# Masked attention of a three-stage kernel: q and k split and hashed in pairs of heads, the exponential before the casts, and VectorE taking the next row extreme before the remainders

## The reference

```
mask = q_bucket[..., :, None] == k_bucket[..., None, :]
scores = where(mask, q @ k.T / sqrt(64), -1e9)
attn = exp(scores - rowmax); attn /= sum(attn) + 1e-9
x = attn @ v                                   # (1536, 512) over both batches
P = sinkhorn(x @ w_gate)                       # 8 experts, soft
x = sum_e P[:, e] * (relu(x @ w1[e]) @ w2[e])  # every token, every expert
out[n] = gate[n] * (relu(x[n] @ v1[e(n)]) @ v2[e(n)])   # one expert for each token
```

## Time and profile before

| | us |
|---|---|
| median of 3 runs (lowest, highest) | 1681.65 (1680.28, 1683.01) |
| the profiled execution | 1685.06 |
| span of its core | 1683.4 |

### The profile page before, as it was taken

How to read it: one execution, slowest core, us unless ns; L and a number is a source line. 1 busy time by engine, 2 the same in 40 slices (tenths; PEclk the granted TensorE clock), 3 DMA queues, 4 the chain that set the end, 5 groups by cost and what they waited for, 6 DMA issues and landing times.

```text
span 1683.4 us, 21614 instructions
## 1 busy us (share of the span) xinstructions
PE 1592.0 (95%) x7588; PEld 1311.0 (78%) x7589; DVE 666.2 (40%) x1227; ACT 505.3 (30%) x943; POOL 305.0 (18%) x380
## 2 busy tenths in 40 slices
PE   7999998899999999999999999999999991789997
PEld 6888887688888888888888888888888871667775
DVE  7999998442211211211311311221122144554223
ACT  5887877311111110111111111111112133553123
POOL 3333342400020120030030030030030004422102
PEclk9999999999999999999999999999999995899999
DMA  4343343200110110110110020020020015653310
GB/s 137 92 122 91 107 122 124 101 1 1 50 51 0 51 50 0 50 50 0 50 50 0 12 88 0 0 100 0 0 87 14 1 51 178 228 204 130 116 40 22
DMA packets 49381, 108.07 MB, mean 64 GB/s; under 512 B 7350, under 2 KB 13494, under 8 KB 49344
## 3 DMA queue, kind: packets, MB, share of 16 engines
q1 hardware_dynamic: 44208, 96.30, 17.2%
q0 software_dynamic: 2400, 6.31, 1.0%
q10 hardware_dynamic: 2736, 4.98, 1.0%
HBM read 81.58 MB, written 13.40 MB: 56 GB/s over the span
## 4 chain that ended last, share of the span: by engine, by line
PE 80%; DVE 7%; issue 5%; ACT 3%; DMA 3%; POOL 2%; DVEq 0%; POOLq 0%; ACTq 0%; SPq 0%
PE psum L352 24%; PE psum L354 24%; PE psum L353 23%; PE psum L575 2%; DVE pt_lo L1075 2%; DVE row_max L1085 1%; DMA w_raw<-in_moe_w_dram 1%; PE psum L527 1%; ACT prob L851 1%; DMA out_dram<-y_row,idx_now 1%; PE psum L789 1%; PE psum L564 1%; ACT pt_hi L844 1%; PE psum L565 1%; PE psum L588 1%
## 5 line engine op out<-in xcount | busy, mean ns | idle before, releaser
L941 ACT ACTIVATE h_hi<-psum 128x512 fp32r<-128x512 f32 x192 | 115.1, 599 | 867.2 <-PE psum L354 867.2
L352 PE MATMUL psum<-xt_lo,w_hi 128*128 128x512 f32 x768 | 303.9, 396 | 0.0
L354 PE MATMUL psum<-xt_hi,w_lo 128*128 128x512 f32 x768 | 301.0, 392 | 0.0
L352 PE MATMUL psum<-w_lo,h_hi 128*128 128x512 f32 x768 | 300.0, 391 | 0.0
L354 PE MATMUL psum<-w_hi,h_lo 128*128 128x512 f32 x768 | 299.3, 390 | 0.0
L353 PE MATMUL psum<-w_hi,h_hi 128*128 128x512 f32 x768 | 298.8, 389 | 0.0
L353 PE MATMUL psum<-xt_hi,w_hi 128*128 128x512 f32 x768 | 298.8, 389 | 0.0
L1246 DVE SCALAR_TENSOR_TENSOR h_lo<-psum,h_hi 128x512 fp32r<-128x512 f32 x192 | 132.8, 692 | 362.0 <-ACT h_hi L941 362.0
L1289 DVE SCALAR_TENSOR_TENSOR tok<-psum,route,tok 128x512 f32<-128x512 f32 x84 | 57.5, 745 | 383.7 <-PE psum L354 383.7
L378 POOL CAST w_hi<-w_raw 128x512 fp32r<-128x512 f32 x64 | 39.3, 615 | 804.1 <-PE psum L354 803.9
L354 PEld LDWEIGHTS psum<-xt_hi,w_lo 128*128 128x128 f32 x768 | 144.2, 188 | 33.5
(11 more groups left out here) (227 smaller groups left out, 2026.5 us busy)
## 6 DMA issues: line engine op xcount, KB each, us to landing
w_raw<-in_moe_w_dram SPq DMA_DIRECT2D x32, 2048.0 KB, 8.2
k_hh<-k_t SPq DMA_DIRECT2D x32, 192.0 KB, 3.9
x_sorted<-zeros SPq DMA_DIRECT2D x21, 257.0 KB, 4.1
x_row<-x_sorted ACTq DMA_DIRECT2D x19, 256.0 KB
k_raw<-in_k_dram SPq DMA_DIRECT2D x16, 192.0 KB, 2.4
q_raw<-in_q_dram SPq DMA_DIRECT2D x16, 192.0 KB, 2.5
v_raw<-in_v_dram SPq DMA_DIRECT2D x16, 192.0 KB, 3.6
k_b<-k_t SPq DMA_DIRECT2D x16, 192.0 KB, 4.2
```

Source lines behind the costliest of these rows:

```text
L352: pe.matmul(acc, a[0], b[1], start=start, stop=False)
L354: return pe.matmul(acc, a[1], b[0], start=False, stop=stop)
L941: act.activation(h_s[0][:, f, :], psum[:, f % 4, :], ACT.Relu).then_inc(m1.h_hi, 1)
```

## The change

The whole change is in attention:
- q and k reach the kernel laid out as [pair of heads, 2 x 64 values, 768 tokens] (the host only reorders them), so turns and their copies are gone; one pair of heads is split at a time, in four pieces over the first four steps of a 12-step round on GpSimd. q is multiplied by minus the score scale there.
- One hash product serves a pair: 8 matmuls for each half of the columns, on TensorE at steps 4 and 5 of a round, and VectorE makes 128x384 bits of each. Eight DMAs a head (six 64-row moves, two of 32 rows of bits) build the score operands.
- Scores run three steps ahead (g+3) in place of two. Because q is negated, VectorE finds a row minimum; the scale and bias of the exponential and the denominators' small addition go to GpSimd.
- Outputs: a matmul with `fold` (two identities side by side) turns the block and adds its halves at once; VectorE scales it from PSUM into `x_nat`. ScalarE's copy of it and GpSimd's two operations are gone.
- ScalarE's order in a step: exponential of g+1, output copy, casts of g. VectorE's order: row minimum of g+3, remainders of g, outputs, hash bits, inverses.

The diff, cut to its core:

```diff
+        i, r = divmod(kk, 2 * IT)
+        return [(r - IT + 2, it + i + 1)] if r in (IT - 2, IT - 1) and known(it, 2 * IT * (it + i + 1)) else []
...
+    def move_k(dma, u):
+
+        rows = slice(u * D, u * D + D)
+        for dst, src in ((k_hh[u][0:D, :], k_hi), (k_hh[u][D:P, :], k_hi), (k_b[u][0:D, :], k_lo)):
+            dma.dma_start(dst.bitcast(F32), src[rows, :].bitcast(F32)).then_inc(s_moved[u], 16)
...
+        def split_qk(i, r):
+
+            lower, upper = slice(0, HALF), slice(HALF, S)
+            if r == 0:
+                for u in range(2):
+                    pool.wait_ge(s_moved[u], 128 * i)
+                pool.wait_ge(s_k_in, 16 * i + 16)
+                copy(k_hi[:], k_raw[:]).then_inc(s_qk_hi, 1)
+                pool.wait_ge(s_qk_hi, 2 * i + 1)
+                pool.tensor_tensor(k_lo[:, lower], k_raw[:, lower], k_hi[:, lower].bitcast(F32), ALU.subtract)
+            if r == 1:
+                pool.tensor_tensor(k_lo[:, upper], k_raw[:, upper], k_hi[:, upper].bitcast(F32),
+                                   ALU.subtract).then_inc(s_qk_split, 1)
...
+        def row_terms(it, u, t):
+
+            g = IT * (2 * it + u) + t
+            c = slice(t % 2, t % 2 + 1)
+            pool.wait_ge(s_min, g + 1)
+            pool.sem_inc(s_pool_go, 1)
+            pool.tensor_scalar(row_scale[:, c], row_min[:, c], BIG / 2, -1.0, ALU.is_lt, ALU.mult)
+            pool.tensor_scalar(row_bias[:, c], row_min[:, c], BIG / 2, row_min[:, c], ALU.is_lt,
+                               ALU.mult).then_inc(s_bias, 1)
+
+        def denominators(it, u, half):
+            hn = 2 * (2 * it + u) + half
+            c = slice(u * IT + 3 * half, u * IT + 3 * half + 3)
+            pool.wait_ge(s_exp, 3 * hn + 3)
+            pool.sem_inc(s_pool_go, 1)
+            pool.tensor_scalar(row_den[:, c], row_sum[:, c], 1e-9, None, ALU.add).then_inc(s_den, 1)
+
+        def step(it, kk):
+            g = 2 * IT * it + kk
+            if known(it, g + 3):
+                row_terms(*at_step(it, kk, 3))
+            if kk % 3 == 0 and known(it, g - 3):
+                i, u, t = at_step(it, kk, -3)
+                denominators(i, u, t // 3)
+            i, r = divmod(kk, 2 * IT)
+            if r < 4 and known(it, 2 * IT * (it + i + 1)):
+                split_qk(it + i + 1, r)
+            if kk % IT == IT - 1 and known(it, g + 1):
+                i, u = divmod(kk // IT + 1, 2)
+                split_v(it + i, u, first=isinstance(g, int) and g < IT)
...
+        def hash_pair(i, half, bank):
+
+            if half == 0:
+                pe.wait_ge(s_qk_split, 2 * i + 2)
+                if isinstance(i, int) and i == 0:
+                    pe.wait_ge(s_k_proj, 8)
+            a = slice(half * HALF, (half + 1) * HALF)
+            for w, parts in ((proj_w[0], (q_lo, q_hi)), (proj_w[1], (k_lo, k_hi))):
                 for part in (1, 0):
-                    mm = pe.matmul(psum[:, bank, 0:HALF], w[part][:], src[:, half * HALF:(half + 1) * HALF],
-                                   start=(w is proj_w[0] and part == 1), stop=(w is proj_w[1] and part == 0))
+                    for src in parts:
+                        mm = pe.matmul(psum[:, bank, 0:HALF], w[part][:], src[:, a],
+                                       start=(w is proj_w[0] and part == 1 and src is q_lo),
+                                       stop=(w is proj_w[1] and part == 0 and src is k_hi))
...
-                tr = pe.transpose(psum[:, 7, j * P:(j + 1) * P], o_t[:, j * P:(j + 1) * P], ident[:])
-            tr.then_inc(s_o_nat, 1)
+                mm = pe.matmul(psum[:, 7, j * D:(j + 1) * D], o_t[:, j * P:(j + 1) * P], fold[:], start=True, stop=True)
+            mm.then_inc(s_o_nat, 1)
...
-            pieces = preparation(it, kk)
             if known(it, g):
                 turn_probs(g, kk % 2)
-            if kk % 3 == 0 and known(it, g - 6):
-
-
-                if known(it, IT * (n + 1)):
-                    pe.wait_ge(*((s_qk_ready, 4 * n + 8) if kk % IT == 0 else (s_bits, 2 * n + 4)))
-                turn_outputs(it, kk)
-            if len(pieces) == 2:
-                prepare(*pieces[0])
-            if known(it, g + 2):
-                scores(*at_step(it, kk, 2))
-            if pieces:
-                if kk % 3 == 0 and known(it, g - 6):
-                    i, u, t = at_step(it, kk, -6)
-                    pe.wait_ge(s_o_copied, 2 * (2 * i + u) + t // 3 + 2)
-                elif kk % IT == 3:
-                    pe.wait_ge(s_bits, 2 * n + 4)
-                prepare(*pieces[-1])
+            if known(it, g + 3):
+                scores(*at_step(it, kk, 3))
+            for half, i in preparation(it, kk):
+                if half == 1:
+                    pe.wait_ge(s_bits, 2 * i + 1)
+                elif known(it, g - 7):
+                    pi, pu, pt = at_step(it, kk, -7)
+                    pe.wait_ge(s_x, 2 * (2 * pi + pu) + pt // 3 + 1)
+                hash_pair(i, half, 7)
             if known(it, g - kk % 3 - 3):
                 values(it, kk)
...
+            if kk % 3 == 0 and known(it, g - 6):
+                if kk % (2 * IT) == IT and known(it, g + IT):
+                    pe.wait_ge(s_bits, 2 * (it + kk // (2 * IT)) + 4)
+                turn_outputs(it, kk)
...
         def step(it, kk):
             g = 2 * IT * it + kk
+            if known(it, g + 1):
+                exp(*at_step(it, kk, 1))
+            if kk % 3 == 0 and known(it, g - 6):
+                copy_outputs(it, kk)
             if known(it, g):
                 hi(it, kk)
-            if kk % 3 == 0 and known(it, g - 6):
-                copy_rows(it, kk)
-            pieces = [piece for piece in preparation(it, kk) if piece[0] != "hash"]
-            if len(pieces) == 2:
-                copy_piece(*pieces[0])
-            if known(it, g + 1):
-                exp(*at_step(it, kk, 1))
-            if pieces:
-                copy_piece(*pieces[-1])
-            if kk % 3 == 2 and known(it, g - 5):
-                copy_outputs(it, kk)
...
-            dve.tensor_reduce(row_max[:, c], psum[:, 2 * (t % 2):2 * (t % 2) + 2, 0:HALF], AX.XY, ALU.max).then_inc(s_max, 1)
-            dve.wait_ge(s_max, g + 1)
-
-            dve.tensor_scalar(row_scale[:, c], row_max[:, c], -BIG / 2, SCALE, ALU.is_gt, ALU.mult).then_inc(s_scale, 1)
-            dve.wait_ge(s_scale, g + 1)
-            dve.scalar_tensor_tensor(row_bias[:, c], row_max[:, c], -1.0, row_scale[:, c], ALU.mult,
-                                     ALU.mult).then_inc(s_bias, 1)
-
+            dve.tensor_reduce(row_min[:, c], psum[:, 2 * (t % 2):2 * (t % 2) + 2, 0:HALF], AX.XY, ALU.min).then_inc(s_min, 1)
+
+        def hash_bits(half, i, bank=7):
+            dve.wait_ge(s_proj, 2 * i + half + 1)
+            dve.tensor_scalar(bits[:, half * HALF:(half + 1) * HALF], psum[:, bank, 0:HALF], thr_mul[:, 0:1],
+                              thr_mul[:, 1:2], ALU.is_gt, ALU.mult).then_inc(s_bits, 1)
...
+        def outputs(it, u, half):
+
+            hn = 2 * (2 * it + u) + half
+            c = u * IT + 3 * half
+            dve.wait_ge(s_o_nat, hn + 2)
+            dve.wait_ge(s_inv, hn + 1)
+            dve.tensor_tensor(x_nat[:, it, 3 * half:3 * half + 3, u * D:(u + 1) * D],
+                              psum[:, 7, 0:3 * D].rearrange("p (t d) -> p t d", d=D),
+                              row_inv[:, c:c + 3].unsqueeze(2).to_broadcast([P, 3, D]), ALU.mult).then_inc(s_x, 1)
...
+            if known(it, g + 3):
+                row_terms(*at_step(it, kk, 3))
             if known(it, g):
                 lo(it, kk)
-            if known(it, g + 2):
-                row_terms(*at_step(it, kk, 2))
-            for piece in preparation(it, kk):
-                if piece[0] == "hash":
-                    hash_bits(*piece[1:])
-            if kk % 3 == 0 and known(it, g - 3):
-                i, u, t = at_step(it, kk, -3)
+            if kk % 3 == 0 and known(it, g - 6):
+                i, u, t = at_step(it, kk, -6)
+                outputs(i, u, t // 3)
+            for half, i in preparation(it, kk):
+                hash_bits(half, i)
+            if kk % 3 == 1 and known(it, g - 4):
+                i, u, t = at_step(it, kk, -4)
                 inverses(i, u, t // 3)
...
+        if name in ("q", "k"):
+            nb, nh, ns, nd = a.shape
+            a = a.reshape(nb * nh // 2, 2, 128, ns // 128, nd).transpose(0, 1, 4, 3, 2).reshape(nb * nh // 2, 2 * nd, ns)```

Three places show the new order. Names end in the number of a buffer; "waits" lists the semaphores, and `row_max` or `row_min` is the extreme that `row_terms` takes. First VectorE in the 12-step loop, before: a step with nothing but its two remainders, the row maximum and its terms, and the start of the next step.

```order
L1075 TENSOR_TENSOR pt_lo_129<-psum,pt_hi_127 128x3x128 [waits pt_hi_a]
L1075 TENSOR_TENSOR pt_lo_129<-psum,pt_hi_127 128x3x128 [waits pt_hi_b]
L1084 REGISTER_ALU
```

(59 more changed lines are left out.)

274 lines of the change are left out of this document (108 added, 166 removed).

## The result

| | before | after |
|---|---|---|
| median us (runs) | 1681.05 (4) | 1722.86 (4) |
| lowest to highest | 1680.28 to 1683.01 | 1719.56 to 1725.01 |
| profiled execution (span) | 1685.06 (1683.4) | 1719.56 (1717.8) |

Ratio 1.0244, 95% interval 1.0230 to 1.0259: slower by 42 us. The forecast was 1723.

What follows compares the result with a forecast made beforehand. VectorE's full list was taken as the bound before the change, a ring of waits after it. Attention's steps +41.1, start +1.5 and end -1.5 on the median 1681.65 gave 1722.8 us, range 1705 to 1742.

Steps and rivals of the forecast that it cites:

- The ring: In attention, scores of g+3, row minimum, remainders of g, next turn wait in a cycle: 3.33 us a loop step.
- The start: Before the first scores: wider splits, 16 hash matmuls, no turns or copies; between -2 and +4 us, +1.5 taken.
- Hash steps: Eight hash matmuls on TensorE lengthen a pair's hash steps: net 0.3 to 0.8 us a pair, 0.45 taken.
- The end: From last attention turn to the mixture's first, copy and two GpSimd operations go: 0 to -3 us, -1.5 taken.
- Hidden work: Hash bits, outputs and inverses fit VectorE's 1.4 us gap; GpSimd's scaling and row terms are hidden too: no cost.
- The clock: TensorE's granted clock in attention stays at 1.00, 2.4 GHz, despite new gaps of 0.9 us a step.
- rival B: TensorE's clock falls to half rate in a third of attention's steps: +54, 1777 us; chance 0.05.
- Rival A: In attention, GpSimd's row terms, the moves or q's split for the hash are late: +14, 1737 us; chance 0.08.
- Rival C: Faster: remainders in attention are not held and TensorE bounds a step at 2.52 us: 1648 us; chance 0.06.

Runs made afterwards that it cites:

- e9: e5 with the moves of the second head's operands issued behind the first head's bits, and two small loads ahead of the moves; 1644.32 us, ratio 0.9777.
- e10: e9 with 30 transposes without use on TensorE ahead of the first hash; 1644.19 us, ratio 0.9777.
- e1: The changed kernel with VectorE doing the remainders of g before the row minimum of g+3; 1678.83 us, ratio 0.9997.
- e3: The changed kernel with TensorE's values' product moved between the turn and the scores; 1780.60 us, ratio 1.0595.
- e5: The changed kernel with remainders first on VectorE and row scale and bias back on VectorE; 1648.84 us, ratio 0.9816; once more 1645.74 us, ratio 0.9784.
- e6: e1 with ScalarE's casts of g ahead of the exponential of g+1; 1835.64 us, ratio 1.0923.
- e4: The changed kernel with row scale and bias on VectorE behind the row minimum, not on GpSimd; 1748.42 us, ratio 1.0412.

## Why the prediction was right, point by point

- **The ring.** Right in place and parts: 0.68, 0.69, 0.98, 0.88 against 0.68, 0.77, 0.99, 0.90 taken. The turn was mis-sized most, by 0.08: I joined the loop's 0.68 with the 0.77 of another, unrolled step, whose own first part was 0.61. From first remainder to scores it was 1.38 there, and it is 1.37 here; the scores follow the second remainder, and the parts must be taken from one step. The step is 3.23, just under the low end of 3.24. I had given unrolled steps 3.26; they are 3.23 too, but for the first (4.18, at a granted clock of 0.50). The ring alone was forecast 7.8 us too long over 93 steps; with the first step and the hash steps it is 4.8: first to last turn forecast 314.7, measured 309.9.
- **The start.** Forecast +1.5, within -2 and +4; measured +9.0. This is the term that failed, and it nearly cancels the 4.8 and the end. Of the 9.0, 6.6 lie ahead of the first scores (22.19 against 15.62) and 2.5 between them and the first turn. Two causes of the first part are seen in the trace after. The 16 hash matmuls went to a TensorE that had been idle for 7.79 us, at 0.32 us each, twice the 0.175 of the loop (the profile's clock column still reads 1.00 here; from 22 to 30 us it reads 0.50, with the same 0.32):

```profile
11.69 0.52 PE L577 MATMUL psum<-q_hi,proj_q_lo 128*128 128x384 f32 x1
...
12.01 0.52 PE L577 MATMUL psum<-q_lo,proj_q_hi 128*128 128x384 f32 x1
```

and the chain of waits runs through DMA issues on SyncE, stretched to 1.7 and 2.0 us, to bits that land 3.5 us after their issue:

```profile
11.25 1.73 SPq L274
...
15.66 1.99 SPq L343
...
17.75 0.85 SPq L285
...
18.65 3.50 DMA k_b<-bits
```

The earlier trace rows had 0.57 for an issue and 2.3 from the bits' last issue to the scores; here it is 22.19 - 18.65 = 3.54. I carried them over as if the twelve moves ahead of them were not there. e9 and e10 took 2.5 and 1.8 us off the start. The second part I had not counted at all. A third block of scores now stands ahead of the first turn: it waits for the first exponential (1.69 us of idle time) and the turn starts 1.49 us after that exponential's end, where before it was 0.14. The clock is at 0.50, so that scores to extreme takes 1.69 and not 0.99, and the row terms come 0.4 us later from GpSimd. No run takes the third block or the lower clock away: in e10 first scores to first turn are still 5.57 us (18.00 to 23.57), at 0.50, against 3.59 before.
- **Hash steps.** Forecast +0.45 a pair, in 0.3 to 0.8; measured 3.80 + 3.44 + 3.11 - 3 x 3.23 = +0.66.
- **The end.** Forecast -1.5, measured -1.63, and 2.14 more behind it, not foreseen: the 32 turns of the mixture's input take 3.71 us against 6.30. It is the clock. Before, TensorE had been idle for 3.70 us ahead of them, and the granted clock was 0.50 from 302 to 306 us; after, it had been idle for 1.26 and the clock is 1.00. The gain is not a sure one: in e1, e3 and e5, behind as short an idle time, the clock falls inside this stretch and it takes 5.1 us.
- **Hidden work.** Outputs (0.35), bits (0.67) and inverses cost nothing, as said. GpSimd's scaling took 2.16 us against at most 2.04, and the row terms 0.53 against 0.4; the half microsecond of slack before the hash was used up, for 1.6 us of waits in all from 60 to 300 us.
- **The clock.** Stayed at 1.00 in the ring, with TensorE busy 17.68 of 20 us and gaps of 0.3 to 0.9 us in a step; rival B did not come. It was no empty rival: the clock fell twice in e1 and five times in e6, behind longer waits (0.64 and 1.65 us; 1.6 to 1.8). That is what the Trainium skill ("TensorE: Matmul & The Clock Gate", section "HAM oscillation — how this bites in real kernels") warns of, waits between bursts of matmuls that send the gate back to half rate; the traces of e1 and e6 agree in that, and in the ring of the kernel after none of it is seen.
- **Rival A** did not come at 3.2 us a step; e1 shows that it comes at 2.1. **Rival C** is refuted for this order, and its sum, 2.52 a step and 1648 us, is what e5 reaches: 2.46 and 1646 to 1649.

The mechanism is right and shown (e1 takes it away, e3 and e4 lengthen it by what they put in). That the total came out to within a microsecond is luck: 4.8 too much in the steps, 7.5 too little at the start, 2.1 unforeseen at the end.
